# Routed scatter that adds to the output's rows, with separate loads for gates, scatter rows and gather rows

## The reference

```python
out = x.copy()
do_compute = x @ w_skip > 0
xc = x[do_compute]
e_idx = argmax(xc @ w_gate, axis=1)          # one of 8 experts for each row
gate_w = softmax(xc @ w_gate)[own e_idx]
for e in range(8):                           # rows of expert e only
    y[mask] = gate_w[mask, None] * (relu(xc[mask] @ w1[e]) @ w2[e])
out[do_compute] = xc + y
```

## Time and profile before

| what | us |
|---|---|
| median of 3 runs | 677.93 |
| lowest and highest | 672.1, 678.08 |
| the profiled execution's own time | 676.7 |
| its span in the profile | 675.1 |
| PE busy in the span | 629.4 (93%) |
| POOL busy in the span | 134.0 (20%) |

### The profile page before, as it was taken

How to read it: one execution, slowest core, us unless ns; L and a number is a source line. 1 busy time by engine, 2 the same in 40 slices (tenths; PEclk the granted TensorE clock), 3 DMA queues, 4 the chain that set the end, 5 groups by cost and what they waited for, 6 DMA issues and landing times. The chain is left out here.

```text
span 675.1 us, 9826 instructions
## 1 busy us (share of the span) xinstructions
PE 629.4 (93%) x3410; PEld 558.7 (83%) x3411; DVE 300.2 (44%) x784; ACT 247.3 (37%) x518; POOL 134.0 (20%) x190
## 2 busy tenths in 40 slices
PE   4799999999999999999999999999969999889892
PEld 4688999898989898989999989898847877678772
DVE  5665556533412134412144344546645365631850
ACT  4764545431301031201032213223335565733761
POOL 6460000000000000000000020211334455524551
PEclk9899999999999999999999999999988999889997
DMA  8814144003400003400013320514574473850740
GB/s 257 264 39 118 46 119 143 16 1 126 126 0 1 1 19 107 124 0 0 0 62 94 109 79 0 156 63 128 129 242 140 165 258 110 282 188 18 255 145 21
DMA packets 41409, 70.06 MB, mean 104 GB/s; under 512 B 13926, under 2 KB 18534, under 8 KB 41376
## 3 DMA queue, kind: packets, MB, share of 16 engines
q1 hardware_dynamic: 37040, 60.73, 29.4%
q0 software_dynamic: 4336, 8.91, 3.6%
HBM read 64.14 MB, written 8.47 MB: 108 GB/s over the span
## 5 line engine op out<-in xcount | busy, mean ns | idle before, releaser
L630 ACT ACTIVATE ht_hi<-ps_h 128x384 fp32r<-128x384 f32 (+1 forms) x104 | 48.6, 467 | 240.0 <-PE ps_h L1007 231.2
L1007 PE MATMUL ps_h<-xt_hi,w_hi_a 128*128 128x384 f32 (+1 forms) x400 | 131.2, 328 | 1.2 <-DVE ht_lo L822 1.2
L1007 PE MATMUL ps_h<-xt_hi,w_lo_a 128*128 128x384 f32 (+1 forms) x400 | 129.5, 324 | 0.0
L1007 PE MATMUL ps_h<-xt_lo,w_hi_a 128*128 128x384 f32 (+1 forms) x400 | 129.4, 324 | 0.0
L1007 PE MATMUL ps_y<-w_hi_a,ht_hi 128*128 128x512 f32 x288 | 115.6, 401 | 0.3 <-POOL w_lo_a L425 0.3
L1007 PE MATMUL ps_y<-w_hi_a,ht_lo 128*128 128x512 f32 x288 | 112.7, 391 | 0.0
L1007 PE MATMUL ps_y<-w_lo_a,ht_hi 128*128 128x512 f32 x288 | 112.5, 391 | 0.0
L822 DVE SCALAR_TENSOR_TENSOR ht_lo<-ps_h,ht_hi 128x384 fp32r<-128x384 f32 (+1 forms) x104 | 54.7, 526 | 118.5 <-ACT ht_hi L630 118.2
L1007 PEld LDWEIGHTS ps_h<-xt_hi,w_hi_a 128*128 128x128 f32 x400 | 75.4, 188 | 2.1 <-DVE ht_lo L822 1.8
L716 DVE TENSOR_TENSOR w_lo_a<-raw,w_hi_a 128x1024 fp32r<-128x1024 f32 x56 | 68.3, 1243 | 18.0 <-ACT w_hi_a L565 17.9
L1007 PEld LDWEIGHTS ps_h<-xt_lo,w_hi_a 128*128 128x128 f32 x400 | 75.4, 188 | 0.4
(11 more groups left out here) (156 smaller groups left out, 859.6 us busy)
## 6 DMA issues: line engine op xcount, KB each, us to landing
raw<-u SPq DMA_DIRECT2D x64, 512.0 KB, 4.6
raw<-w SPq DMA_DIRECT2D x32, 512.0 KB, 4.1
vt<-v SPq DMA_DIRECT2D x17, 256.0 KB, 2.9
kt<-k SPq DMA_DIRECT2D x8, 384.0 KB, 4.7
qz<-q SPq DMA_DIRECT2D x18, 128.0 KB, 3.6
x_rows<-x POOLq DMA_DIRECT2D x9, 256.0 KB, 4.7
out<-x POOLq DMA_DIRECT2D x9, 256.0 KB, 4.9
kt<-k SPq DMA_DIRECT2D x1, 256.0 KB, 3.6
```

Source lines behind the costliest of these rows:

```text
L630: a.activation(ht_hi[:, pos, 0:P * tiles], ps_h[:, pos % 2, 0:P * tiles], ACT.Relu).then_inc(h_hi_done, 1)
L1007: ins = mm(dst, hi_lo[l], rhs_hi_lo[r], start=(first and n == 0), stop=(last and n == 2))
```

## The change

The scatter of a slot no longer writes x plus y. It carries `compute_op=ALU.add`, so the DMA adds `y_gated` to the rows of `out`, where x is already stored. With that `x_kept`, `y_out`, `add_x` and all of POOL's copies in `around` go, and so does the memset of `x_kept`. The three users of the records get loads into buffers of their own: `ids` for the gather, `gate_ids` for ACT's gate, `out_ids` for the scatter. The gates' and scatter's records are loaded from `lists` again, one slot later, at a row kept in registers. `around(s)` now first sends out the finished slot s-3 (`finish_slot`), loads the gate records of slot s-2, the gather records of slot s, and the scatter records of slot s-2, and then waits for the turn of slot s-1 and gathers slot s. ACT's `y_gated` waits for the scatter before and for its own gate records. At the start one gather goes out in place of two, and one scatter to nobody in place of two. PE, DVE and SP run the same instructions as before. Each turn of `around` issued a gather, a scatter and one load of 1 KB; now it issues a gather, a scatter and three loads of 1 KB.

The diff, cut to its core (declarations of tiles and semaphores left out):

```diff
@@ gpsimd, preparation
-            g.iota(ids_out[:], pattern=[[0, 2]], base=NOBODY, channel_multiplier=0).then_inc(ids_made, 1)
-            pool.wait_ge(ids_made, 1)
-            g.memset(y_out[:], 0.0).then_inc(ys_added, 1)
-            pool.wait_ge(ys_added, 1)
-            g.memset(xg[:], 0.0).then_inc(ys_gated, 1)
+            g.memset(y_gated[:], 0.0).then_inc(ys_gated, 1)
             pool.wait_ge(ys_gated, 1)
+            g.memset(xg[:], 0.0).then_inc(xg_clear, 1)
...
-                if t == NT - 1:
-                    g.memset(x_kept[:], 0.0).then_inc(x_kept_clear, 1)
-                    pool.wait_ge(x_kept_clear, 1)
@@ gpsimd, helpers
-            def add_x():
-                g.tensor_tensor(y_out[:], y_gated[:], x_kept[:], ALU.add)
-                g.tensor_copy(ids_out[:], ids_kept[:]).then_inc(ys_added, 1)
             def scatter():
-                g.indirect_dma_start(out=out, out_offset=bass.IndirectOffsetOnAxis(ids_out[:, 0:1], 0),
-                                     in_=y_out[:], in_offset=None, bounds_check=N - 1,
-                                     oob_is_err=False).then_inc(scattered, 16)
+                g.indirect_dma_start(out=out, out_offset=bass.IndirectOffsetOnAxis(out_ids[:, 0:1], 0),
+                                     in_=y_gated[:], in_offset=None, bounds_check=N - 1, oob_is_err=False,
+                                     compute_op=ALU.add).then_inc(scattered, 16)
+            def finish_slot():
+                pool.wait_ge(out_stored, 16 * NT)
+                pool.wait_ge(out_ids_landed, landed)
+                pool.wait_ge(ys_gated, nth)
+                scatter()
+                own = nc.s_assert_within(pool.snap(own_row), 0, E2 * LIST - P)
+                pool.wait_ge(listed, 16 * NT)
+                load_ids(gate_ids, own, gate_ids_landed)
+                return own
             def around(s, row):
-                pool.reg_mov(nth, s)
-                pool.reg_mov(later, s + 1)
-                pool.reg_mov(landed, 16 * s)
+                pool.reg_mov(nth, later)
+                pool.reg_mov(later, s)
+                pool.reg_mov(landed, landed_later)
+                pool.reg_mov(landed_later, 16 * s)
+                own = finish_slot()
                 pool.wait_ge(listed, 16 * NT)
-                pool.wait_ge(xs_ready, nth)
-                g.tensor_copy(ids_moved[:], ids[:]).then_inc(ids_free, 1)
-                pool.wait_ge(listed, 16 * NT)
-                pool.wait_ge(ids_free, nth)
-                load_ids(ids, row)
+                pool.wait_ge(xg_landed, landed)
+                load_ids(ids, row, ids_landed)
                 pool.wait_ge(listed, 16 * NT)
                 pool.wait_ge(scattered, landed)
-                pool.wait_ge(ys_gated, nth)
-                add_x()
-                pool.wait_ge(listed, 16 * NT)
-                pool.wait_ge(ys_added, nth)
-                g.tensor_copy(x_kept[:], xg[:])
-                g.tensor_copy(ids_kept[:], ids_moved[:]).then_inc(xg_kept, 1)
-                pool.reg_mov(landed, 16 * s + 16)
+                load_ids(out_ids, own, out_ids_landed)
                 pool.wait_ge(x_stored, 16 * NT)
-                pool.wait_ge(xg_kept, nth)
-                pool.wait_ge(ids_landed, landed)
-                gather(xg, ids, xg_landed)
-                scatter()
+                pool.wait_ge(xs_ready, later)
+                pool.wait_ge(ids_landed, landed_later)
+                gather()
+                pool.reg_mov(own_row, row_after)
+                pool.reg_mov(row_after, row)
@@ gpsimd, start of the routed stage
-            load_ids(ids_kept, 0)
-            load_ids(ids, row_1)
+            load_ids(ids, row_1, ids_landed)
+            load_ids(out_ids, E2 * LIST, out_ids_landed)
             pool.wait_ge(x_stored, 16 * NT)
-            pool.wait_ge(ids_landed, 32)
-            gather(x_kept, ids_kept, x_kept_landed)
-            gather(xg, ids, xg_landed)
-            pool.wait_ge(out_stored, 16 * NT)
-            pool.wait_ge(ids_made, 1)
-            scatter()
-            scatter()
...
+            pool.wait_ge(ids_landed, 16)
+            gather()
@@ gpsimd, end
-            pool.wait_ge(scattered, total)
-            pool.wait_ge(ys_gated, later)
-            add_x()
-            pool.wait_ge(listed, 16 * NT)
-            pool.wait_ge(xg_landed, landed)
-            pool.wait_ge(ys_added, later)
-            scatter()
...
+            own = finish_slot()
+            pool.wait_ge(listed, 16 * NT)
+            pool.wait_ge(xg_landed, landed)
+            pool.wait_ge(scattered, landed)
+            load_ids(out_ids, own, out_ids_landed)
+            pool.wait_ge(out_stored, 16 * NT)
+            pool.wait_ge(out_ids_landed, landed_later)
+            pool.wait_ge(ys_gated, later)
+            scatter()
@@ scalar, slot
-                act.wait_ge(ys_added, s + 1)
-                act.wait_ge(xg_kept, s + 1)
+                act.wait_ge(scattered, 16 * s + 16)
+                act.wait_ge(gate_ids_landed, 16 * s + 16)
                 act.wait_ge(ys_ready, s + 1)
-                a.activation(y_gated[:], ps_y[:, 0, :], ACT.Copy, scale=ids_kept[:, 1:2].bitcast(F32)
+                a.activation(y_gated[:], ps_y[:, 0, :], ACT.Copy, scale=gate_ids[:, 1:2].bitcast(F32)
```

More of the change, by code:

```diff
@@ L203, in build_block @@
         ids = sb("ids", [P, 2], U32)
[L204 to L207, removed]
+        gate_ids = sb("gate_ids", [P, 2], U32)
+        out_ids = sb("out_ids", [P, 2], U32)
+        sb("unused_b", [P, 64])
         xg = sb("xg", [P, D])
-        y_out = sb("y_out", [P, D])
+        y_gated = sb("y_gated", [P, D])
         with ExitStack() as dense:
@@ L235, in build_block @@
         hs_lo = sb("hs_lo", [P, FC, P], F32R)
-        x_kept = sb("x_kept", [P, D])
-        y_gated = sb("y_gated", [P, D])
         ps_h = psum("ps_h", [P, 2, 512])
@@ L248, in build_block @@
         zeroed, zeroed_more = sem("zeroed"), sem("zeroed_more")
-        masks_made, ids_made, made = sem("masks_made"), sem("ids_made"), sem("made")
+        masks_made, xg_clear, made = sem("masks_made"), sem("xg_clear"), sem("made")
         keys_landed = [sem("keys_landed_a"), sem("keys_landed_b"), sem("keys_landed_c")]
@@ L447, in _ @@
             landed = pool.alloc_register("landed")
+            landed_later = pool.alloc_register("landed_later")
             next_row = pool.alloc_register("next_row")
[L449 to L454, removed]
-                g.indirect_dma_start(out=dst[:], out_offset=None, in_=x_rows,
-                                     in_offset=bass.IndirectOffsetOnAxis(rows[:, 0:1], 0), bounds_check=N - 1,
-                                     oob_is_err=False).then_inc(landed, 16)
@@ new lines, in _, with load_ids, gather @@
+            row_after = pool.alloc_register("row_after")
+            def load_ids(dst, row, landed):
+                pool.dma_start(dst[:], lists[bass.ds(row, P), :]).then_inc(landed, 16)
+            def gather():
+                g.indirect_dma_start(out=xg[:], out_offset=None, in_=x_rows,
+                                     in_offset=bass.IndirectOffsetOnAxis(ids[:, 0:1], 0), bounds_check=N - 1,
+                                     oob_is_err=False).then_inc(xg_landed, 16)
+            def scatter():
+                g.indirect_dma_start(out=out, out_offset=bass.IndirectOffsetOnAxis(out_ids[:, 0:1], 0),
+                                     in_=y_gated[:], in_offset=None, bounds_check=N - 1, oob_is_err=False,
+                                     compute_op=ALU.add).then_inc(scattered, 16)
@@ L507, in _ @@
             row_1 = nc.s_assert_within(pool.snap(next_row), P, LIST)
+            pool.reg_mov(own_row, 0)
+            pool.reg_mov(row_after, row_1)
+            pool.reg_mov(later, 1)
+            pool.reg_mov(landed_later, 16)
             pool.wait_ge(listed, 16 * NT)
[L509 to L510 removed]
+            load_ids(ids, row_1, ids_landed)
+            load_ids(out_ids, E2 * LIST, out_ids_landed)
             pool.wait_ge(x_stored, 16 * NT)
[L512 to L525 removed]
+            pool.wait_ge(ids_landed, 16)
+            gather()
             with pool.If(first_slots > 1):
@@ L542, in _ @@
             pool.reg_mov(nth, slots)
+            pool.reg_mov(landed, 16 * slots)
             pool.reg_mov(later, slots + 1)
-            pool.reg_mov(landed, 16 * slots)
-            pool.reg_mov(total, 16 * slots + 16)
-            pool.wait_ge(listed, 16 * NT)
-            pool.wait_ge(scattered, total)
-            pool.wait_ge(ys_gated, later)
-            add_x()
+            pool.reg_mov(landed_later, 16 * slots + 16)
+            own = finish_slot()
             pool.wait_ge(listed, 16 * NT)
             pool.wait_ge(xg_landed, landed)
-            pool.wait_ge(ys_added, later)
+            pool.wait_ge(scattered, landed)
[3 more added lines that the diff above has]
+            pool.wait_ge(ys_gated, later)
             scatter()
-            pool.reg_mov(landed, 16 * slots + 32)
```

(2 more changed lines are left out.)

13 lines of the change are left out of this document (5 added, 8 removed).

## The result

The changed kernel takes 668.7 us (median of 22 executions), the kernel before 675.0 on the same chips (22 executions). The ratio is 0.9907, 95% interval 0.9887 to 0.9926: about 0.9% faster. The forecast was 662, its range 654 to 670: the time lies inside the range, but the gain is 6.3 us where 16 were forecast. 3 us of that forecast gain lay in the median of the three runs shown (677.93), which was high; from profile to profile (676.7 to 669.3) the gain is 7.4 where the sum said 14.8.

The account below looks back on a forecast made before the run. The prediction took PE, busy 93% of the span, as the bound, held up by late gathers in the routed stage. Its terms, 5.5 + 3.0 + 4.8 + 1.3 + 0.2 = 14.8 us off 676.7, gave 662, range 654 to 670.

Parts of the forecast that it names:

- Term 1: Start of the routed stage: first gather leaves earlier, stall falls from 6.6 to 2.5 us, less clock loss; gain 5.5 us.
- Term 2: Turns at 522.34 and 548.90: their waits for the gather, 1.35 and 1.68 us, go; gain 3.0 us.
- the weights aren't pressed: Claim within Term 2: the next slot splits nothing, so no wait for weights eats the 3.0 us.
- Term 3: Turns at 576.00 and 593.09: gather stalls go, but 2.4 us return as a wait for weights; gain 4.8 us.
- Term 4: Turns at 633.55 and behind: one stall returns as a wait for weights, part of the rest is saved; gain 1.3 us.
- The 1.59: Within Term 4: the 1.59 us stall ahead of the turn at 633.55 returns ahead of the hidden turn.
- half of 2.4: Within Term 4: of the other 2.4 us lost, weight pieces freed earlier give back about half, put at 1.3.
- Term 5: The end: last scatter leaves 1.5 us sooner after y_gated, adding costs 1.3 us more landing; net gain 0.2 us.
- Rival A: The weight feed takes nearly all: Term 3 and Term 4 give 2.8 us together, time 668; chance 0.16.
- Rival B: The weights don't bind and the clock stays at 1.00: time about 654.6; chance 0.08.
- Rival C: The adding scatter's landing paces POOL's loop: today's mean at 10.3 us, about 701 at 13; chance 0.10.

Follow-up runs that it names:

- a1: The changed kernel unaltered, timed again: 668.3 us.
- a2: The changed kernel with a plain scatter that overwrites in place of adding, so the addition of x is left out: 664.3 us.
- b3: The kernel before with two edits: the scatter adds, and POOL copies y_gated in place of adding x: 667.7 us.
- c2: b3 without x_kept and its gather, with slot 1's records loaded first: 663.9 us.
- c3: b3 with a plain scatter in place of the adding one, so the addition of x is left out: 665.7 us.
- e3: c2 with the last scatter sent straight from y_gated: 662.8 us.
- b1: The changed kernel with a plain scatter, a second gather of the x rows in each slot, and DVE adding x: 666.5 us.
- b2: The changed kernel with a plain scatter, a second gather of the x rows in each slot, and POOL adding x: 688.1 us.
- a3: The changed kernel with all scatters sent to rows out of bounds, leaving out the routed rows' update: 662.9 us.

## Why the prediction was wrong

The step that failed is the price of the adding scatter. The forecast had it as a longer landing, 1.3 us once, at the end, and as nothing in the steady loop. The runs showed 4.3 us in the 11 slots (147.7 in a1, 143.4 in a2) and 2.1 at the end by the profiles, and 3.6, plus or minus 2.6, for the whole by six executions of each. Two further terms were off for other reasons: the landing of the first records, and a stretch behind the last landing.

**Term 1, the start (5.5 forecast, 2.2 measured).** The order was right, the landing of the record load was mis-sized: 5.7 us for 4.1, on top of 1.1 us later issue, so the gather left 2.7 late. It then landed in 5.0. The stall was 4.15 and not 2.5, and the clock behind it cost 2.9, as much as behind 6.63. The term is unsteady: in a1, the same kernel, the records landed in 5.1, the stall was 2.8, and the first hidden turn came 7.95 us after the turn, so the clock cost 1.6, just what I had allowed. Its first turn came 3.0 us earlier than before and the slot behind was 1.3 shorter than before's without its stall (14.12 for 15.43), 4.3 together. Yet its profiled execution took 668.5, because there the slot of 15.77 took 17.10 and that of 12.37 took 12.97.

**Term 2 (3.0 forecast, 1.9 measured).** The stalls went. But "the weights aren't pressed" failed: 3.65 us lie between second hidden turn and turn at 519.51, where a clean slot has 2.76, and 544.80 comes after 12.92. The second is the adding scatter's doing (12.36 in a2). The first isn't: a2 has 3.45 in that place, a1 2.95.

**Term 3 (4.8 forecast, 5.2 measured).** Right, and by its steps: 40.7 us for three slots where 41.0 were forecast, a hidden turn that waits 2.65 for 2.4. It was in part luck: in a1 the same three slots took 41.9, a term of 3.9.

**Term 4 (1.3 forecast, 0.1 measured).** The 1.59 came back as forecast, ahead of the hidden turns. The "half of 2.4" (which is 1.2, not 1.3) given back by earlier weights was taken by the scatter in the same DMA engines: 13.96 for the slot ahead of the turn at 624.12, 12.36 in a2.

**Term 5, the end (+0.2 forecast, -2.0 measured).** 1.5 saved, as said. Landing was 1.8 longer, not 1.3, and 1.8 more lie behind the landing (7.9 for 6.1), which no term had. That stretch isn't the adding's: it is 7.9 or 8.0 wherever a turn of POOL's loop issues five DMAs and the last landing is on record, with adding or without (a2: 661.6 less 651.12 and 2.6), 6.0 or 6.1 where it issues three (before, b3, c2, c3, e3), and 8.9 where it issues six (b1, b2). So it grows with the DMAs of the program, but no run varied their number alone, and the trace has no instruction there; what it is stays open.

**The sum.** 2.2 + 1.9 + 5.2 + 0.1 - 2.0 = 7.4. By size the start missed most in this profile, 3.3 us, but in a1 only 1.2; terms 2, 4 and 5 missed alike in both. Without the adding (a2) the profile gains 13.5 on that of before (675.1 less 661.6), near the 14.8, so in sum the rest of the forecast nearly held; by the medians a2 gains 11.2. The Trainium skill's rule ("Collectives: The Full Stack", The bandwidth ceiling), two source reads for each byte, was given as a longer landing only. A landing was the smaller part: 4.4 us against 3.2 by the estimate from that page and "DMA: Bandwidth & Descriptors", and the traces show three times the time in the engines (2.1 against 0.64 us of all 16 for 128 rows), more than a doubling of reads gives. I counted the adding scatter by its latency, priced at the end, and not by what it does to the loads behind it.

**The rivals.** Rival A named that traffic and the time, 668, but by another split: it took terms 3 and 4 down to 2.8, and they gave 5.3, while the end, which it left at nothing, took 2.0. That its time came within 1 us was in part luck. Rival B fell with the clock at the start and the waits for weights. Rival C needed landings of 10.3 us; they were 3.0 to 7.8.

**Was the early gather needed?** b3 says no: the stalls were POOL's add and copies by 1 to 2 us, and it takes 667.7, as the changed kernel does, with its first stall still 6.4. The change paid for its early gather with a scatter in a worse place (by the profiles, 4.3 us of adding in the 11 slots where b3 and c3 show none) and a longer end.

## What to carry to other kernels

Price a DMA by the time that it holds the DMA engines as well as by its landing, and look at which loads its data will meet there. Where a wait is 2 us long, look first for 2 us on the path that feeds it before the order is rebuilt: two lines did it here. And where executions lie 5 us apart, an effect of 3 us needs both the medians and the place in the trace.

## What the runs showed of the hardware

An adding scatter of up to 128 rows of 2 KB took POOL 1.59 to 1.67 us to issue in quiet (plain 1.0) and landed in 4.4 to 4.9 us (plain 2.6 or 2.7); one with next to no rows, issued at 561.25, landed in 3.0. With 128 rows it held the DMA engines 2.1 us at 115 GB/s (plain 0.64 at 410). The whole queue q0 from 485 us on, with the same 4.16 MB, had 4128 packets and 12.1% of the engines' time when adding, 3296 and 7.3% when not (a2). A scatter whose rows are all out of bounds (a3, adding form) took the same 1.65 us of POOL, and its semaphore 2.8 us.

Copies of 128x2 on POOL took 0.18 us or 0.7 to 1.3, of 128x512 0.61 or 1.0 to 1.5, in one and the same kernel. The traces of before, b3 and c3 have 45 long ones in the routed stage, and 44 of them ran, at least in part, while DVE made the low part of a weight piece (`w_lo`, both inputs in SBUF); of the 117 short ones 20 did. No run moved the one against the other alone, so the link is seen and not tested.
